# Strassen's scheme for the first layer of a feed-forward over pairs of token tiles, on one Trainium2 core

## The reference

```python
for t in range(S):          # q, k, v: batch 4, heads 8, S = 768, D = 64
    state = gamma * state + k_t v_t^T          # per head
    y[t] = scale * q_t @ state
x = y.transpose(0, 2, 1, 3).reshape(3072, 512)
# first feed-forward: w_in 512 x 1024, w_out 1024 x 512
h = x @ w_in
sm = exp(h - max(h)) / (sum(exp(h - max(h))) + 1e-9)
solu = h * sm
ln = (solu - mean) / sqrt(var + 1e-6) * g_ln
x = ln @ w_out
# second feed-forward: w_in 512 x 2048, w_out 2048 x 512
h = x @ w_in
out = (h * cos(h)) @ w_out
```

## Time and profile before

| | |
|---|---|
| median of 3 runs | 895.1 us (894.12 to 895.19) |
| the profiled execution | 894.13 us, of which its span is 892.3 us |
| TensorE busy | 884.3 us, 99% |
| VectorE busy | 588.7 us, 66% |
| ScalarE busy | 436.9 us, 49% |
| GpSimd busy | 148.0 us, 17%, all of it before 380 us |
| first stage, one tile | about 16 us |

### The profile page before, as it was taken

The page is one execution under the profiler, slowest core; times in us unless marked ns, Lnnn a source line. Parts: engine busy times, 40 slices in busy tenths (PEclk is TensorE's granted clock), DMA queues, the critical chain, the costliest instruction groups (busy, mean ns, idle before and its releaser), DMA issues.

```text
span 892.3 us, 14480 instructions
## 1 busy us (share of the span) xinstructions
PE 884.3 (99%) x5218; PEld 773.4 (87%) x5218; DVE 588.7 (66%) x849; ACT 436.9 (49%) x663; POOL 148.0 (17%) x186
## 2 busy tenths in 40 slices
PE   8999999999999999999999999999999999999998
PEld 6788888888888888889999999999999999999997
DVE  5865777577756777576666765566756658755654
ACT  2533433343334433465545755455655547564553
POOL 2332435234342442400000000000000000000000
PEclk9999999999999999999999999999999999999999
DMA  9534665456645563649854447344365434454301
GB/s 339 195 125 143 208 214 177 145 200 222 218 148 180 173 235 131 225 136 343 292 167 114 121 133 255 108 125 122 109 191 184 129 108 126 119 180 124 108 0 71
DMA packets 106662, 148.18 MB, mean 166 GB/s; under 512 B 7424, under 2 KB 77184, under 8 KB 106624
## 3 DMA queue, kind: packets, MB, share of 16 engines
q1 hardware_dynamic: 106624, 147.69, 51.6%
HBM read 112.01 MB, written 35.65 MB: 165 GB/s over the span
## 4 chain that ended last, share of the span: by engine, by line
PE 96%; DVE 1%; DMA 1%; SPq 1%; issue 0%; ACT 0%; POOL 0%; POOLq 0%; ACTq 0%
PE bank L318 28%; PE bank L321 28%; PE bank L320 28%; PE bank L557 3%; PE bank L642 2%; PE bank L606 2%; PE bank L589 2%; PE bank L677 2%; PE bank L577 1%; DMA w_raw<-w_in 1%; DVE w1i_l L1090 0%; DVE w1o_l L1095 0%; DMA out<-o_a 0%; SPq L419 0%; DVE nmax L1101 0%
## 5 line engine op out<-in xcount | busy, mean ns | idle before, releaser
L318 PE MATMUL bank<-yc_h,ring 128*128 128x384 f32 x448 | 151.5, 338 | 0.0
L320 PE MATMUL bank<-yc_l,ring 128*128 128x384 f32 x448 | 151.3, 338 | 0.0
L321 PE MATMUL bank<-yc_h,ring 128*128 128x384 f32 x448 | 150.9, 337 | 0.0
L1184 DVE SCALAR_TENSOR_TENSOR gg<-turns,c 128x768 f32<-128x768 int32 x64 | 61.0, 954 | 63.8 <-ACT turns L849 63.8
L855 ACT ACTIVATE gg<-gg 128x768 f32<-128x768 f32 x64 | 54.1, 846 | 80.2 <-DVE gg L1191 80.1
L849 ACT ACTIVATE turns<-c 128x768 int32<-128x768 f32 x64 | 54.2, 846 | 79.1 <-DVE c L1254 76.6
L318 PEld LDWEIGHTS bank<-yc_h,ring 128*128 128x128 f32 x448 | 84.2, 188 | 7.9 <-issue 0.5
L320 PEld LDWEIGHTS bank<-yc_l,ring 128*128 128x128 f32 x448 | 84.2, 188 | 7.2
L321 PEld LDWEIGHTS bank<-yc_h,ring 128*128 128x128 f32 x448 | 84.1, 188 | 0.0
L318 PE MATMUL bank<-w1i_h,x_h 128*128 128x512 f32 x192 | 77.8, 405 | 1.2 <-DVE w1i_l L1090 0.9
L318 PE MATMUL bank<-w1o_h,z_h 128*128 128x512 f32 x192 | 77.1, 401 | 0.0
(11 more groups left out here) (101 smaller groups left out, 1724.5 us busy)
## 6 DMA issues: line engine op xcount, KB each, us to landing
ring<-w_split SPq DMA_DIRECT2D x224, 256.0 KB, 2.8
w_split<-w_out SPq DMA_DIRECT2D x16, 896.0 KB, 4.2
w2o_split<-wo_out SPq DMA_DIRECT2D x16, 512.0 KB, 4.6
w2o<-w2o_split SPq DMA_DIRECT2D x8, 1024.0 KB, 8.4
raw<-qT SPq DMA_DIRECT2D x24, 256.0 KB, 3.0
raw<-kT SPq DMA_DIRECT2D x24, 256.0 KB, 2.7
raw<-kn SPq DMA_DIRECT2D x24, 256.0 KB, 3.7
raw<-vn SPq DMA_DIRECT2D x24, 256.0 KB, 4.8
```

The costliest lines, as they stand in the source:

```text
L318: eng.matmul(dst, ah, bh, start=first and i == 0, stop=False, skip_group_check=read_between)
L320: eng.matmul(dst, ah, bl, start=False, stop=False, skip_group_check=read_between)
L321: m = eng.matmul(dst, al, bh, start=False, stop=last_one and i == n - 1, skip_group_check=read_between)
L1184: dve.scalar_tensor_tensor(gg[:, r, :], turns[:, r, :], -TWO_PI_HI, flat(c_32[:, r, :, :]), ALU.mult, ALU.add)\
```

## The change

- The first layer (h = x @ w_in) is computed for a pair of tiles by Strassen's scheme: x of two tiles is a 2 x 2 block matrix (tile x half of the 512 inner columns), w_in is another (half of the inner rows x half of the 1024 columns), and seven products of blocks with two 128-row parts each replace eight. TensorE's parts `PA` (P1, P2), `PB` (P6, P5), `PC` (P7) and `PD` (P3, P4) are run over two steps, around T0 and T1: odd steps have PA and PB, even ones PC and PD.
- Two PSUM banks (`bank_x`, `bank_y`) take the products. Intermediate results are copied out by ScalarE (`f_a`, `f_b`), and the four quarters of h (h11, h12, h21, h22) are put together in SBUF: three by additions on VectorE, h21 by a copy on ScalarE. The maximum (`ME`, `MO`), the exponential, U and the squares then read h from SBUF.
- x is copied to `xs` in 32-bit form (`X`), four sums are made on GpSimd (`XS`), the high halves of seven operands on ScalarE (in `X` and `XH`), the low halves on VectorE (`XE`, `XL`).
- The seven weight operands are made from w_in at the start: four sums of 128 x 1024 on GpSimd (`TS`), high halves on ScalarE (`WVH`), low halves on VectorE (`WVL`). w_out's conversion moves from the first lists to step 4 (`WOH`, `WOL`), and its first unit is loaded after the others, once w_in's sums are made.
- The copy of y transposed (`YT`) moves from VectorE to ScalarE.
- Lags grow by two (`LAG` from 4 to 6), and the tail's order is rewritten.

The core of the diff:

```diff
-STEP = [("PK", 0), ("PV", 0), ("SG", 1), ("WE", 1), ("L1a", 2), ("T0", 3), ("L1b", 2),
-        ("T1", 3), ("EX", 2), ("OS", 1), ("SC", 0), ("DL", 1), ("OP", 1), ("YT", 4), ("U", 2), ("SM", 0), ("X", 1),
-        ("ST", 1), ("WS", 0), ("L2a", 3), ("SQ", 2), ("L2b", 3), ("CEN", 2),
-        ("VAR", 2), ("WH", 0), ("WD", 0)]
-LAG = 4
+STEP = [("PK", 0), ("PV", 0), ("SG", 1), ("WE", 1), ("MO", 4), ("PA", 3), ("PC", 4), ("T0", 5),
+        ("PB", 3), ("PD", 4), ("ME", 4), ("T1", 5), ("EX", 4), ("OS", 1), ("SC", 0), ("DL", 1),
+        ("OP", 1), ("YT", 6), ("U", 4), ("SM", 0), ("X", 1), ("XE", 1), ("ST", 1), ("XS", 1),
+        ("WS", 0), ("L2a", 5), ("SQ", 4), ("XH", 1), ("L2b", 5), ("CEN", 4), ("XL", 1), ("VAR", 4),
+        ("WH", 0), ("WD", 0)]
+LAG = 6
...
+        pe_first = [("Z", 11), ("SC", 0), ("Z", 4), ("OP", 0), ("DL", 0), ("Z", 2), ("SC", 1),
+                    ("OS", 1), ("OP", 1), ("DL", 1), ("PA", 0), ("SC", 2), ("OS", 2), ("DL", 2),
+                    ("OP", 2), ("PB", 0), ("SC", 3)]
+        act_first = [("WVH", 0), ("X", 0), ("WVH", 1), ("X", 1), ("PA", 0), ("WVH", 2), ("XH", 1),
+                     ("WVH", 3), ("WVH", 4), ("X", 2), ("PB", 0), ("WVH", 5), ("WVH", 6)]
+        dve_first = [("QS", 0), ("ID", 0), ("SC0", 0), ("SC1", 0), ("QS", 1), ("ST", 0),
+                     ("WVL", 0), ("XE", 0), ("SC0", 1), ("SC1", 1), ("ST", 1), ("WVL", 1),
+                     ("WVL", 2), ("PA", 0), ("SC0", 2), ("SC1", 2), ("XL", 1), ("WVL", 3),
+                     ("ST", 2), ("WVL", 4), ("XE", 2), ("WVL", 5), ("WVL", 6), ("SC0", 3),
+                     ("SC1", 3)]
+        pool_first = [("NS", 0), ("NS", 1), ("TS", 0), ("SG", 1), ("XS", 1), ("QS", 2), ("NS", 2),
+                      ("TS", 1), ("SG", 2), ("QS", 3), ("NS", 3)]
+        outputs = {"U": 0, "ST": 1, "CEN": 2, "VAR": 3}
...
+                if n == 4 and name in outputs:
+                    head += [("WOH", outputs[name]), ("WOL", outputs[name])]
...
+                    if u == KD:
+                        sp.wait_ge(w1i_lo, ORDER.index(P6) + 1)
+                        sp.wait_ge(ws_done, 4)
...
+            def l1(b, t, p):
+
+                m = t // 2
+                if isinstance(b, int) and b * TILES + t == 0:
+                    pe.wait_ge(w1i_lo, ORDER.index(p) + 1)
+                if p == P1:
+                    pair_wait(pe, xa_lo, b, m)
+                    pair_wait(pe, h21_done, b, m - 1)
+                elif p == P2:
+                    pair_wait(pe, h12_done, b, m - 1)
+                elif p == P6:
+                    pair_wait(pe, xs_lo, b, m)
+                    pair_wait(pe, f1_done, b, m)
+                elif p == P5:
+                    pair_wait(pe, h11_done, b, m)
+                elif p == P7:
+                    pair_wait(pe, f2_done, b, m)
+                elif p == P3:
+                    pair_wait(pe, f5_done, b, m)
+                else:
+                    pair_wait(pe, h22_done, b, m)
+                x, w = XPART[p], ORDER.index(p)
+                products(pe, bank_y if p in (P2, P5, P3) else bank_x, [
+                    (xv_h[:, x, k, :], xv_l[:, x, k, :], w1i_h[:, w, k, :], w1i_l[:, w, k, :])
+                    for k in range(2)], p in (P1, P2, P5), True, True).then_inc(l1_done, 1)
...
+                elif name == "PA" and par == 0:
+                    l1_wait(dve, b, m, P2)
+                    pair_wait(dve, f1_done, b, m)
+                    wait(dve, sq1_done, b, t - 2)
+                    dve.tensor_tensor(h_of[0][:, 0:512], bank_y, f_a[:, :], ALU.add)\
+                        .then_inc(h11_done, 1)
+                elif name == "PC" and par == 0:
+                    l1_wait(dve, b, m, P7)
+                    pair_wait(dve, f5_done, b, m)
+                    wait(dve, sq1_done, b, t - 1)
+                    dve.tensor_tensor(h_of[1][:, 512:1024], bank_x, f_a[:, :], ALU.add)\
+                        .then_inc(h22_done, 1)
```

More of the change, by code:

```diff
@@ L78 @@
 LO, HI = 0, 1
+XA11, XA12, XA21, XA22, XS1, XS2, XS3, XS4 = range(8)
+XPART = {P1: 0, P2: 1, P4: 2, P5: 3, P6: 4, P7: 5, P3: 6}
+ORDER = (P1, P2, P6, P5, P7, P3, P4)
+PAIRS_IN = TILES // 2
+PAIRS_ALL = NT // 2
 FILL = [[], [(HI, 0)], [(HI, 1)], [(HI, 2), (HI, 3), (HI, 4)], [(HI, 5)],
@@ L280, in wait @@
+        for n in range(NT, NT + LAG):
+            for name, behind in STEP:
+                if n - behind < NT and name not in ("WE", "WS", "WH", "WD"):
+                    tail.append((name, n - behind))
+                tail += late.get((n, name), [])
+        tail += [("Q", P2)]
         def wait(eng, s, batch, tile, per=1, i=0, per_batch=TILES):
@@ L293, in wait_state, with pair_wait, l1_wait @@
                  per_batch=TILES - 1)
+        def pair_wait(eng, s, batch, pair, per=1, i=0):
+            wait(eng, s, batch, pair, per, i, per_batch=PAIRS_IN)
+        def l1_wait(eng, batch, pair, p):
+            pair_wait(eng, l1_done, batch, pair, 7, ORDER.index(p))
         def wait_decay(eng, s, batch, tile):
@@ L434, in _ @@
             load_nv(2, 2)
-            for u in range(KD, W1_UNITS):
+            for u in range(KD + 1, W1_UNITS):
                 load_w1(u)
+            load_w1(KD)
             load_next(1, 0)
@@ L469, in tile @@
                     load_next(t, (n + 2) % RAW)
-                store_yt(t - LAG)
-            sp.wait_ge(w1_lo, W1_UNITS)
-            for n in range(LAG, TILES):
+                if not isinstance(t, int) or t >= LAG:
+                    store_yt(t - LAG)
+            sp.wait_ge(w1i_lo, 7)
+            for n in range(4, TILES):
                 tile(0, n)
@@ L586, in step @@
                     wait(pe, q_sc, b, t)
[L587 removed]
+                    wait(pe, x_done, b, t - 1)
                     for p in range(PAIRS):
@@ L809, in step @@
                         .then_inc(y_done, 1)
+                elif name == "YT":
+                    wait(act, yt_done, b, t)
+                    if isinstance(b, int) and t in yt_of:
+                        wait(act, t_done, b, NT - 1, 2, 1)
+                        act.copy(yt_of[t], ps_t[:, :]).then_inc(ytc_done, 1)
+                        return
+                    if not isinstance(b, int) or t > 0:
+                        act.wait_ge(y_stored, 16 + b * (16 * TILES) + 16 * t)
+                    act.copy(yt32, ps_t[:, :]).then_inc(ytc_done, 1)
                 elif name == "SQ":
                     wait(act, nmu_done, b, t)
-                    act.activation(e_b, u_b, ACT.Square, bias=nmu[:, par:par + 1],
+                    act.activation(e_b, h_of[par], ACT.Square, bias=nmu[:, par:par + 1],
                                    accum_out=ssq[:, par:par + 1]).then_inc(sq1_done, 1)
```

327 lines of the change are left out of this document (188 added, 139 removed), and 8 rows, old and new, of tables (dve_first, pe_first).

## The result

| | time, median of 4 (range) | ratio to before, 95% interval |
|---|---|---|
| before | 894.91 us (894.12 to 895.19) | |
| after | 981.17 us (977.70 to 984.61) | 1.0965 (1.0925 to 1.1006) |

The change makes the kernel 86 us slower. The forecast was 929 us, range 901 to 946: the direction was right, the size was not. The profiled execution took 981.93 us, of which 980.1 are the span. Of all the executions in this document one, of experiment 4, fell in a slower state of the chip and is left out of its row.

What follows compares the result with a forecast made beforehand. TensorE, busy 884.3 of 892.3 us, was taken as the bound. 892.3 - 16.5 (matmuls) + 31.8 (stalls) + 19 (start) + 1 (tail) = 927.6 span; with 1.8 around it 929 us, range 901 to 946.

Steps and rivals of the forecast that it cites:

- -16.5 us for the matmuls: TensorE, first layer: 6 fewer 512-column matmuls a pair, 72 in all at 0.229 us, saving 16.5 us.
- 9 x 2.4 + 6 x 1.7: Middle: nine odd-step stalls of 2.4 us and six even-step stalls of 1.7 us, +31.8 us (bounds 5.7 and 46).
- Even step: P4 waits for VectorE's h22 addition; VectorE free at S+4.4 (S: first layer's start), stall 1.7 us (bounds 0.5, 2.6).
- Odd step: P5 waits for VectorE's h11 addition behind weight pair and maximum; stall 2.4 us (bounds 0.3 and 3.4).
- Rival 4: Longer chain, WS delaying the weight cast: stalls 3.4 and 2.6, start +26, tail +2, about 950 us; 20% for above 936.
- The granted clock should stay at 2.4 GHz: TensorE, whole run: full clock kept despite new waits, as through the waits of the earlier trace.
- fourth SC about 36: Start, forecast +19 us (bounds +8, +26): fourth SC, attention's q and k product, at about 36 us, after 39.34 before.
- all four sums (about 30.7): Start: SP waits for GpSimd's four 1024-column sums until about 30.7 us before the last w_out load.
- P, Q of the second feed-forward still fill it: Tail: TensorE still filled by the second feed-forward's work, so the tail costs +1 us (0 to 5).
- Rival 1: VectorE in time at P5 and P4, no stall, start only +8: 887 us, faster; 12%.
- Rival 2: GpSimd out of the way, bare durations in the middle, start as replayed: 903 us; 15%.
- Rival 5: Whole kernel: gain and loss cancel, 895 us; 3%.

Runs made afterwards that it cites:

- experiment 4: Kernel after the change, with the copy of y transposed moved back from ScalarE to VectorE: 998.50 us, ratio 1.1157.
- Experiment 6: Experiment 3 with x's copy earlier, maximum behind the additions, y transposes between the second layer's halves, and P6 earlier in the tail: 922.35 us, ratio 1.0310.
- Experiment 2: Kernel after the change, with GpSimd's weight sums (WS) put ahead of its sums of x (XS), nothing else: 961.42 us, ratio 1.0756.
- Experiment 10: Kernel after the change, with the sine table loaded behind the last tile's exponential instead of ahead of it: 978.44 us, ratio 1.0940.
- experiment 5: Kernel after the change, with 62 extra identity matmuls filling TensorE's gaps in the first 80 us: 978.93 us, ratio 1.0923.
- experiment 8: Kernel after the change, with only the start's loads, first casts and w_out conversions reordered: 978.56 us, ratio 1.0944.
- experiment 9: Experiment 6 with start and tail rearranged, among others two w_in sums moved to VectorE and the sine table loaded later: 906.88 us, ratio 1.0132.
- experiment 11: Experiment 9 with the start's low halves, weight casts and w_out casts reordered again: 902.90 us, ratio 1.0097.
- experiment 12: Experiment 11 with pair 0's h22 addition earlier, w_out low halves behind the additions, and 27 idle identity matmuls: 899.12 us, ratio 1.0048.
- experiment 3: Kernel after the change, with all the second feed-forward's weight preparation placed inside the step, not across its end: 944.20 us, ratio 1.0544.

## Why the forecast was right in direction and wrong in size

The profiled execution is 52 us above the forecast: 18 of them in the middle, 15 in the start and 19 in the tail.

**-16.5 us for the matmuls: right.** Experiment 6 shows -13.1 over 18 steps, without any wait of TensorE, where the forecast's pitch gives -12.4.

**The middle, +31.8 forecast, 50.0 measured.** The step was "9 x 2.4 + 6 x 1.7". The places (P5, P4), the count and the cause were as said; T1 does not wait, as said, and h11 does stand behind MO. The waits sum to 41.4 us, inside the forecast's bounds of 5.7 and 46; the rest of the loss is below. The sizes were not right:
- *Even step*, 2.2 us each instead of 1.7, six times, +3. VectorE was free at S+4.8, not at S+4.4: the trio of GpSimd does come earlier, but w_out still takes 1.58 us and wo_out 1.52 beside it. The bound "2.6 as before" was the nearer one.
- *Odd step*, in the first of each batch 1.3 us, in the other two 4.1 (1.3 at P6 and 2.75 at P5): 9 waits at P5 and 6 at P6 sum to 28.3 us, 21.6 forecast. The failing sentence is the replay "the weight pair begins at S+3.1 instead of 1.75, partly repaid by less collision. h11 at S+7.1 to 7.6". XL did end where the replay had it (S+2.2). The weight pair began at S+3.5, because GpSimd's WS behind XS ends only at S+2.5 and ScalarE's WH waits for it. And nothing was repaid: where the replay's times leave 2.2 to 2.7 us for the pair, it took 3.5 us beside GpSimd's work, as long as before, and h11 came at S+8.9. In the first odd step of each batch, where GpSimd's scalings start only behind it, the pair takes 1.09 and 0.69 us. I also followed XS to VectorE and did not follow WS to ScalarE, so I missed what stands behind WH there, f_a, and the wait at P6. Rival 4, which had 20%, names this chain ("WS behind XS and XL delays the weight cast"), with a stall of 3.4. Experiment 2 shows both parts: with WS ahead the waits at P6 vanish, the pair takes 1.6 us, and the kernel gains 19.8 us.
- *The clock.* The three waits of the middle sum to 41.4 us; the loss is 50.0. The other 8.6 are TensorE running slower. "The granted clock should stay at 2.4 GHz" failed. Three stretches of the middle have a granted clock of 0.83 over 10 us, as here, the kernel after, with the P4 wait of 229.45 and P5's of 251.50 just ahead (start and end, length, busy (instructions), granted clock, DMA share, GB/s):

```profile
230.00:240.00 10.00, 10.00 (x82) 0.83 0.54 195
...
250.00:260.00 10.00, 8.50 (x75) 0.83 0.49 162
```

  A third of 10 us at 1.2 GHz gives a mean of 0.83 and costs 1.7 us, so by this estimate three stretches cost some 5 of the 8.6. Experiment 10 measures it: its middle has the same waits (41.5 us), no such stretch, and is 4.5 us shorter. Experiments 5 and 8 have one stretch each and middles of 319.2 and 319.0 us. What then remains, some 4 us, is in part the slower first matmul behind the 15 waits at P4 and P5 (0.34 us to the next instead of 0.23, some 1.7 together); the rest stays unassigned. The waits of the earlier trace rows, on which I had based the sentence, are two, not 21.

**The start, +19 forecast, 33.9 measured.** The step "fourth SC about 36" failed by 8.7 us: it stands at 44.69. Most of that was there already at its own premise, "all four sums (about 30.7)": GpSimd's last sum ends at 37.88, and tile 3's q, loaded behind it, arrives at 43.37. The later steps lost 6 us more, so that step 5 ends at 85.8 and not at 71. My replay had P1 at about 20 (24.94 in fact), SC(2) at about 25 (30.04), T0(0) at 51 (62.32), P6 of pair 1 at 54 (66.53) and P5 at 60 (72.47). What it left out:
- ScalarE's first instruction is the activation table's load. Before, it was over by 2.1 us; now it stands behind the wait for the weights, 14.96 to 16.24, and X(0) ends at 17.8 instead of 16.1.
- I gave VectorE and GpSimd their durations of the middle. In the start both often work at once on operands that lie in SBUF alone. Kernel after, VectorE and GpSimd:

```profile
18.47 2.84 DVE L1206 TENSOR_TENSOR xv_l<-xs,xv_h 128x512 fp32r<-128x512 f32 x1
...
35.57 3.40 DVE L1233 TENSOR_TENSOR w1i_l<-work,w1i_h 128x1024 fp32r<-128x1024 f32 x1
...
42.02 0.68 DVE L1206 TENSOR_TENSOR xv_l<-xs,xv_h 128x512 fp32r<-128x512 f32 x1
...
17.58 3.19 POOL L1139 TENSOR_TENSOR work<-w_raw,work 128x1024 f32<-128x1024 f32 x1 [0.21 <-DMA w_raw<-w_in]
...
34.25 3.63 POOL L1139 TENSOR_TENSOR w_raw<-w_raw,work 128x1024 f32<-128x1024 f32 x1
```

  The same 512-column low half takes 2.84 us beside GpSimd's sum and 0.68 without it, the 1024-column one 3.40 against the 1264 ns of the earlier trace rows. Experiments 9, 11 and 12 moved sums and order (12 also kept TensorE busy with idle matmuls) and brought the start's loss from 33.9 to 17.2 us, no further. Taking the collisions away altogether was not tried, so how much of the 17 us that experiment 12's start still loses is due to them stays open.
- The clock, at 0.76 in this stage, is a small cause: experiment 5 raised it to 0.96, and the start became 3.5 us shorter. The forecast had it at full speed.

**The tail, +1 forecast, 19.8 measured.** The failing sentence is "P, Q of the second feed-forward still fill it". TensorE's waits from 400 to 490 us in the kernel after:

```profile
PE bank L703 <- DVE z_l L1284: 5.7, 4, 1.5
PE bank L680 <- DVE work L1270: 3.2, 1, 3.2
PE bank L361 <- ACT c L1028: 2.3, 1, 2.3
```

L1284 is z_l, for which YT (L703) waits four times and T1 once (2.05 us, not shown); L1270 is CEN, for which T0 waits. Where attention is over, its four groups no longer stand between T1 and YT, and YT waits 1.4 us for each tile's low half; T0 of the last tile waits for CEN; the cosine's c waits for the reloaded table. That is 14.3 us idle, with the rest at a granted clock of 0.94. Experiments 6 and 9 together took the tail's loss from 19.8 to 4.9 us (13.7 after the first).

**The weighing of the rivals.** Rivals 1, 2 and 5 are out. Rival 4 was the nearest in kind, with 3.4 and 2.6 for stalls that were 4.1 and 2.2; but its tail (+2) and its ceiling for the start (+26) were both too low. The range failed in three places: the middle's bounds held its waits but not the clock, the start's upper bound came from durations of the steady state, and the tail's (5) supposed that TensorE would find work there as before.

The Trainium skill (SBUF — State Buffer, "Who interferes with whom") has a VectorE operation with two SBUF inputs and a GpSimd one that reads SBUF lock each other out for a whole instruction. The traces agree: 2.84 us against 0.68 above. The prediction's second reading, that bare durations would return with GpSimd idle, is borne out in experiment 3, where all 16 w_out operations take 1.08 or 1.09 us, and in the first odd step of each batch after. Bare they are 1.09 and 0.69, each 0.14 longer than the prediction had them.

The Trainium skill (ScalarE: Activation LUTs, "What ACT_TABLE_LOAD costs") gives a switch of tables some 1.28 us for the load and about as much again for a drain. The traces show the 1.28, and in the kernel after the next instruction starts at once behind it (454.23 + 1.28, the exponential at 455.52), as the load does behind the one before it (453.38 + 0.83); the drain is not seen here.

## What to carry to other kernels

When a change makes an operation need a result sooner, follow every queue to the end: ask for each instruction ahead of the new one who releases it, and for each instruction behind that one who waits (here GpSimd's WS, ScalarE's WH, and f_a behind it). Where the steady state had all engines in order, the start and the end are where a scheme that needs two tiles at once loses: 22 us remained there after every wait of the middle was gone, against 16 saved. Cost them with the durations that the start itself shows, not with those of the middle. And where one edit is judged by a total that moves by 7 us between executions, read its own stage between two marks: experiment 5's gain is 3.5 us there and 2 in the total.
